# A first expert tile gathered by products with ones, begun beside the ordering of the tiles

## The reference

```python
x = attention(q, k, v)                  # 2 x 8 heads, 768 rows of 64, masked by buckets
P = a0 + a1*h + a2*h**2 + a3*h**3       # h = x @ w_in, 1536 x 2048
y = (P / (1 + |b0|*|h| + |b1|*h**2)) @ w_out
expert = argmax(y @ w_gate)             # 8 experts
gate   = max(softmax(y @ w_gate))
for e in range(8):
    rows = expert == e
    out[rows] = gate[rows] * (relu(y[rows] @ w1[e]) @ w2[e])   # 512 -> 1024 -> 512
```

## Time and profile before

| | us |
|---|---|
| median of three runs | 819.56 |
| lowest and highest run | 818.15, 820.72 |
| the profiled execution: time, and the core's span | 819.36, 817.6 |
| PE busy | 779.0 (95% of the span) |
| DVE, ACT, POOL busy | 564.1, 491.3, 455.6 |
| mean granted TensorE clock | 0.979 |

### The profile page before, as it was taken

The page is one execution under the profiler, slowest core; times in us unless marked ns, Lnnn a source line. Parts: engine busy times, 40 slices in busy tenths (PEclk is TensorE's granted clock), DMA queues, the critical chain, the costliest instruction groups (busy, mean ns, idle before and its releaser), DMA issues.

```text
span 817.6 us, 13322 instructions
## 1 busy us (share of the span) xinstructions
PE 779.0 (95%) x4255; PEld 688.7 (84%) x4255; DVE 564.1 (69%) x967; ACT 491.3 (60%) x973; POOL 455.6 (56%) x404
## 2 busy tenths in 40 slices
PE   6999999999998999999999999994999999999994
PEld 5899899899996889999999999893788888888883
DVE  4788888888896787877788777974454454454451
ACT  4678878878897998778778877944222224223000
POOL 3235265265157688458557644426885659765700
PEclk8899999999999999999999999995999999999998
DMA  9898988985840940950790050074672536460200
GB/s 197 177 209 170 204 173 169 209 168 130 201 148 23 309 160 2 352 176 1 245 375 27 1 206 1 14 259 159 202 239 61 205 133 216 142 234 24 85 14 19
DMA packets 71844, 123.43 MB, mean 151 GB/s; under 512 B 33343, under 2 KB 36127, under 8 KB 67681
## 3 DMA queue, kind: packets, MB, share of 16 engines
q1 hardware_dynamic: 64176, 90.71, 41.3%
q10 hardware_dynamic: 5056, 25.56, 9.4%
q0 software_dynamic: 2544, 6.31, 2.0%
HBM read 60.26 MB, written 34.24 MB: 116 GB/s over the span
## 4 chain that ended last, share of the span: by engine, by line
PE 88%; ACT 5%; DVE 3%; issue 2%; DMA 1%; POOL 1%; SPq 0%; ACTq 0%; POOLq 0%; DVEq 0%
PE ps L1390 7%; PE ps L1478 5%; PE ps L1480 5%; PE ps L1479 5%; PE ps L1512 5%; PE ps L1513 5%; PE ps L1511 5%; PE ps L1656 4%; PE ps L1657 4%; PE ps L1658 4%; PE ps L1682 4%; PE ps L1680 4%; PE ps L1681 4%; PE ps L1378 4%; PE ps L1379 4%; PE ps L1402 4%
## 5 line engine op out<-in xcount | busy, mean ns | idle before, releaser
L786 POOL TENSOR_TENSOR split<-wraw,split 128x512 f32 (+1 forms) x112 | 140.3, 1286 | 54.9 <-ACT split L947 51.4
L947 ACT ACTIVATE split<-wraw 128x512 f32 (+1 forms) x128 | 68.8, 618 | 142.0 <-PE ps L1658 65.9
L1111 DVE TENSOR_TENSOR ptl<-ps,pth 128x512 fp32r<-128x512 f32 x144 | 98.7, 686 | 36.1 <-ACT pth L881 34.1
L761 POOL TENSOR_TENSOR hw<-hw,ha 128x384 f32<-128x384 f32 x64 | 65.4, 1021 | 72.7 <-ACT hw L959 72.7
L881 ACT ACTIVATE pth<-ps 128x512 fp32r<-128x512 f32 x144 | 86.7, 602 | 31.4 <-PE ps L1390 31.3
L1091 DVE TENSOR_REDUCE negmax<-ps 128x1 f32<-128x768 f32 x96 | 91.0, 948 | 8.4 <-PE ps L1379 8.4
L872 ACT ACTIVATE pr<-ps,negmax 128x768 f32<-128x768 f32 x96 | 86.8, 904 | 6.8 <-DVE negmax L1091 6.8
L1390 PE MATMUL ps<-cst,pr 128*128 128x128 f32 x576 | 88.5, 274 | 1.1 <-ACT pr L872 1.1
L1478 PE MATMUL ps<-xh,wih 128*128 128x384 f32 x256 | 86.2, 337 | 1.0 <-DVE hp L1147 1.0
L1480 PE MATMUL ps<-xh,wil 128*128 128x384 f32 x256 | 86.3, 337 | 0.0
L1479 PE MATMUL ps<-xl,wih 128*128 128x384 f32 x256 | 85.9, 336 | 0.0
(11 more groups left out here) (205 smaller groups left out, 2008.9 us busy)
## 6 DMA issues: line engine op xcount, KB each, us to landing
routed<-blank SPq DMA_DIRECT2D x33, 771.0 KB, 13.6
wraw<-in_moe_w ACTq DMA_DIRECT2D x24, 1024.0 KB, 5.4
wraw<-in_moe_w SPq DMA_DIRECT2D x8, 1024.0 KB, 5.4
operand<-qk_hi SPq DMA_DIRECT2D x31, 192.0 KB, 4.2
operand<-qk_hi SPq DMA_DIRECT2D x15, 384.0 KB, 4.7
operand<-qk_lo SPq DMA_DIRECT2D x30, 192.0 KB, 4.3
operand<-mask SPq DMA_DIRECT2D x14, 384.0 KB, 5.0
xg<-routed SPq DMA_DIRECT2D x19, 256.0 KB
```

The costliest lines, as they stand in the source:

```text
L786: pool.tensor_tensor(split_piece(E_LO[x], ring, k), wraw[:, x, i, :], split_piece(E_HI[x], ring, k).bitcast(F32), ALU.subtract).then_inc(e ...
L1111: dve.tensor_tensor(ptl[:, at:at + CW], ps[:, 4 + c % 2, :], pth[:, at:at + CW].bitcast(F32), ALU.subtract).then_inc(ptl_done, 1)
```

## The change

- Blocks 0 to 7 are routed as before. SP then reads slots 0 to 127 back at once (`s_x0`), and POOL's scatters of blocks 8 to 11 wait until that has landed.
- The rows of the blocks 8 to 11 that belong to tile 0 are picked on PE. DVE compares slot numbers with an iota (`picks(j)`), which gives a 128x128 matrix of ones and zeros, and `gather(j)` multiplies the block by it: four matmuls into PSUM bank 5. The read-back rows are added with the identity, four more matmuls, and `xt_ready` is raised.
- `choose` is cut in two: `gate(c)` has the gate values. For c = 2 and 3 it stands later. ACT's turned block 11 comes ahead of exponential 2, and `ranks(2)` ahead of `logit(10)`.
- Four matmuls whose result is not used (`keep_warm(4)`) stand before `gather(9)`.
- ACT copies `xth` of tile 0, between two groups of its weight pieces.
- `mm1` multiplies by `xth` first and by `xtl` after, half by half, and so waits for `xt_hi` only. In tile 0 the last four small products of the ordering stand after its first eight matmuls; `table_done` follows them.
- PE's order for the first tiles: mm1(0), turn_h(0), half of mm2(0), turn_x(1), mm1(1), turn_x(2), the other half of mm2(0), turn_h(1). DVE's follows it.
- `hs` lies ahead of `hth` in memory, an iota of 128 columns is loaded with the constants.

The diff, cut to what the prediction speaks of:

```diff
+            sp.wait_ge(g_done, NSTEP * M4)
+            sp.dma_start(iota[:, :], consts[:, C_IOTA:C_IOTA + P]).then_inc(s_iota, 16)
...
                 sp.dma_start(xg[t % 2][:, :], rows[:, 0:DM]).then_inc(s_xg[t % 2], 16)
+                if t == 1:
+                    sp.wait_ge(xt_ready, 1)
+                    sp.dma_start(gi[:, 0, :], routed[0:P, DM:ROW]).then_inc(s_xg[0], 16)
...
+            sp.wait_ge(s_route, 16 * FIRST_PICK)
+            sp.dma_start(xg[0][:, :], routed[0:P, 0:DM]).then_inc(s_x0, 16)
+            sp.wait_ge(rows_done, 1)
             sp.wait_ge(s_route, 16 * NJ)
-            rows_in(0)
-            sp.wait_ge(rows_done, 1)
...
                 for j in range(CT * c, CT * (c + 1)):
+                    if j == FIRST_PICK:
+                        pool.wait_ge(s_x0, 16)
                     pool.indirect_dma_start(out=routed, ...
...
-            for x in range(2):
-                weights_hi(x, 1, RING_STEP, range(8))
+            weights_hi(0, 1, RING_STEP, range(8))
+            weights_hi(1, 1, RING_STEP, range(4))
+            act.wait_ge(xt_ready, 1)
+            act.activation(xth[:, :, :], ps[:, x_bank(0), :].rearrange("p (k n) -> p k n", n=P), ACT.Copy).then_inc(xt_hi, 1)
+            weights_hi(1, 1, RING_STEP, range(4, 8))
...
+            def picks(j):
+
+                dve.tensor_scalar(pick[:, j - FIRST_PICK, :], iota[:, :], slotf[:, j:j + 1], None, ALU.is_equal).then_inc(pick_done, 1)
...
             choose(2)
             place(2)
+            dve.wait_ge(slot_done, 5)
+            dve.wait_ge(s_iota, 16)
+            picks(8)
+            gate(2)
             choose(3)
             place(3)
+            dve.wait_ge(slot_done, 7)
+            for j in range(9, NJ):
+                picks(j)
...
+            x_in(0)
             dve.wait_ge(seg_pe, 4)
             link(dve.tensor_scalar(tab_need[0:1, :], ...
...
+            relu(0)
+            dve.wait_ge(s_route, 16 * NJ)
+            h_in(0, range(0, 1))
+            x_in(1)
+            h_in(0, range(1, 2))
+            for t in range(1, NSLOT_TILES):
                 relu(t)
...
+            def gather(j):
+
+                pe.wait_ge(pick_done, j - FIRST_PICK + 1)
+                for kt in range(KD):
+                    pe.matmul(ps[:, X0_BANK, kt * P:(kt + 1) * P], y[:, j, kt:DM:KD], pick[:, j - FIRST_PICK, :],
+                              start=(j == FIRST_PICK and kt == 0), stop=False)
+
+            def keep_warm(n):
+
+                some = split_piece(S_W1H, 0, 0)
+                for i in range(n):
+                    pe.matmul(ps[:, 4, :], some[:, 0:P], some, start=True, stop=True)
...
+            ranks(2)
             logit(10)
-            ranks(2)
             logit(11)
+            gather(8)
             ranks(3)
...
+            pe.wait_ge(e_lo[0], 8)
+            keep_warm(4)
+            gather(9)
...
+            pe.wait_ge(s_x0, 16)
+            for kt in range(KD):
+                mm = pe.matmul(ps[:, X0_BANK, kt * P:(kt + 1) * P], xg[0][:, kt:DM:KD], ident, start=False, stop=(kt == KD - 1))
+            mm.then_inc(xt_ready, 1)
...
-                pe.wait_ge(xt_done, t + 1)
+                pe.wait_ge(xt_hi, t + 1)
                 for c in range(2):
                     wait(pe, hs_done, 2 * t - 1 + c)
                     for kt in range(KD):
                         k = KD * c + kt
                         pe.matmul(ps[:, c, :], xth[:, kt, :], weights(S_W1H, t, k), start=(kt == 0), stop=False)
-                        pe.matmul(ps[:, c, :], xtl[:, kt, :], weights(S_W1H, t, k), start=False, stop=False)
-                        mm = pe.matmul(ps[:, c, :], xth[:, kt, :], weights(S_W1L, t, k), start=False, stop=(kt == KD - 1))
+                        pe.matmul(ps[:, c, :], xth[:, kt, :], weights(S_W1L, t, k), start=False, stop=False)
+                    if c == 0:
+                        if t == 0:
+                            last_segments()
+                        pe.wait_ge(xt_done, t + 1)
+                    for kt in range(KD):
+                        mm = pe.matmul(ps[:, c, :], xtl[:, kt, :], weights(S_W1H, t, KD * c + kt), start=False, stop=(kt == KD - 1))
...
-            turn_x(0)
             mm1(0)
+            turn_h(0)
+            mm2(0, range(0, KF // 2))
             turn_x(1)
-            turn_h(0)
             pe.wait_ge(table_done, 1)
-            for t in range(1, NSLOT_TILES):
+            mm1(1)
+            turn_x(2)
+            mm2(0, range(KF // 2, KF))
+            turn_h(1)
+            for t in range(2, NSLOT_TILES):
```

More of the change, by code:

```diff
@@ L248, in build @@
         chosen = put("chosen", [P, E], F32)
+        iota = put("iota", [P, P], F32)
+        pick = put("pick", [P, NJ - FIRST_PICK, P], F32)
         put = Map(csel_at)
@@ L1197, in choose, with gate @@
                     dve.wait_ge(scum_done, j + 1)
+            def gate(c):
+                js = slice(CT * c, CT * (c + 1))
                 dve.wait_ge(ex_done, c + 1)
@@ L1227, in _ @@
             choose(0)
+            gate(0)
             y_add(NSTEP - 1, 0)
@@ L1233, in _ @@
             choose(1)
+            gate(1)
             first_lo_of(1, range(6, 8))
@@ L1254, in _ @@
             dve.scalar_tensor_tensor(out=runs[on, 1:2], in0=upto[on, :], scalar=own(G_TWO), in1=runs[on, 0:1], op0=ALU.is_gt, op1=ALU.add).then_inc(seg_dve, 1)
+            gate(3)
             dve.wait_ge(seg_pe, 1)
@@ L1298, in relu, with h_in @@
                     dve.tensor_scalar(hs[:, c * 512:(c + 1) * 512], ps[:, c, :], 0.0, None, ALU.max).then_inc(hs_done, 1)
-            def h_in(t):
-                for c in range(2):
+            def h_in(t, halves=range(2)):
+                for c in halves:
                     dve.wait_ge(ht_ready, 2 * t + c + 1)
@@ L1617, in _ @@
             pe.matmul(ps[on, 7, 128:128 + NSEG], spread(runs[on, 1:2]), cst[on, C_ID:C_ID + NSEG], start=True, stop=True).then_inc(seg_pe, 1)
+            gather(10)
+            gather(11)
             pe.wait_ge(seg_dve, 2)
@@ L1623, in _, with last_segments @@
             pe.matmul(ps[0:1, 7, 224:224 + NTAB], seg[on, G_RING:G_RING + 1], inside[on, :], start=True, stop=True).then_inc(seg_pe, 1)
[L1624 to L1628 removed]
+            def last_segments():
+                pe.wait_ge(seg_dve, 4)
+                pe.matmul(ps[0:1, 7, 256:256 + NTAB], order[on, 0:1], inside[on, :], start=True, stop=True)
+                pe.matmul(ps[0:1, 7, 288:288 + E], seg[on, G_EXPERT:G_EXPERT + 1], chosen[on, :], start=True, stop=True)
+                pe.matmul(ps[0:1, 7, 288 + E:288 + 2 * E], seg[on, G_RING:G_RING + 1], chosen[on, :], start=True, stop=True)
+                pe.matmul(ps[0:1, 7, 320:320 + E], order[on, 1:2], chosen[on, :], start=True, stop=True).then_inc(seg_pe, 1)
             rings, needs = [0], [8]
@@ L1669, in turn_h, with mm2 @@
                     mm.then_inc(ht_ready, 1)
-            def mm2(t):
-                pe.wait_ge(ht_done, 2 * t + 2)
+            def mm2(t, kts=range(KF)):
+                pe.wait_ge(ht_done, 2 * t + (2 if kts.stop == KF else 1))
                 wait(pe, yo_done, t - 1)
@@ L1676, in mm2 @@
                     pe.wait_ge(e_lo[1], needs[t])
-                for kt in range(KF):
+                for kt in kts:
                     if t == 0:
```

64 lines of the change are left out of this document (34 added, 30 removed).

## The result

The forecast was wrong. Over 20 runs of each, the changed kernel takes 821.59 us in the median (818.04 to 827.52), the kernel before 819.57 (817.70 to 820.72). The ratio is 1.0026 with a 95% interval of 1.0013 to 1.0038: slightly slower, where 816.6 and a range up to 819.4 were forecast. The profiled execution took 820.68 (before 819.36), its span is 818.8, PE is busy for 787.2 us (before 779.0) and the mean granted clock is 0.985 (before 0.979). So PE works more, for the most part at a better clock, and the program does not end earlier.

What follows compares the result with a forecast made beforehand. PE's unbroken work after 580 was taken as the bound, reached through the routing waits. mm1(0) 4.1 us earlier, tile 0 ending 4.7 earlier, less 1.7 for the order, limited by POOL at mm1(3), gave 2.8: 816.6 us, range 812.8 to 819.4.

Steps and rivals of the forecast that it cites:

- the price of the products in front of mm1(0): PE before mm1(0): a gather 1.13 us, read-back products 562.4 to 563.5; with ACT's copy, mm1(0) begins at 564.15, 4.1 earlier.
- The rival in which the clock never falls: From 553 to 562 PE's added products hold the clock: gain 6.8 us, time 812.6, chance 0.13.
- The rest of the front: Before mm1(0): picks 0.3 us each, read-back there by 560.6, later scatters landed at 567.7, ACT's copy 0.60.
- the delay of 0.7: ACT began logit(11) only at 552.05, unexplained; 0.65 us won if that goes, 0.6 taken.
- The end at 572.2: mm1(0) takes 8.1 us from 564.15, clock rising after 4.6 us; the end before was 576.87.
- where 7.1 was taken: From mm1(0)'s end to mm1(1)'s start, through relu, turns, DVE's steps and half of mm2(0): 7.1 us, formerly 2.56.
- The second fall: Rival: clock withdrawn in PE's short work behind mm1(0), costing 5.1 to 5.9 us, time 822.1, chance 0.12.
- The first fall: After routing, the clock falls at 554 while matmuls with 8 to 24 columns run; forecast low up to about 569.
- The sum: At tile 3, mm1(3) begins at 601.3 instead of 604.14: gain 2.8 us, 819.36 to 816.6.
- the 1.7 of the new order: From mm1(0)'s end to mm1(2): 16.6 us instead of 14.9, costing 1.7 of the 4.7 won.
- POOL's 0.3: At mm1(3), POOL's eight pieces of r = 2 ready at 601.3, wanted at 601.15; slack of 7.8 us used up.

Runs made afterwards that it cites:

- the last wait filled: Kernel before plus ten unused matmuls in PE's wait ahead of the last tile's mm2: median 818.28 us, ratio 0.9990.
- the old-order kernel: Changed kernel with the second tile's order as before, mm2(0) in one piece after mm1(1): median 825.94 us, ratio 1.0086 to the kernel before.
- the one with POOL before the table: Changed kernel with POOL's wait for the table moved from the second expert's low parts to the third's: median 837.34 us, ratio 1.0226 to the kernel before.
- the ordering filled: Kernel before plus 37 unused 128x512 matmuls in PE's waits between the last logits and mm1(0): median 821.07 us, ratio 1.0028.

## Why the prediction failed

**The term that was mis-sized.** The forecast missed by 5.0 us. The first step that failed is the price of the products in front of mm1(0): "Into this gap go keep_warm(4), 4 x 0.427 = 1.7, and gather(9), 1.13", then two gathers 2.3 and the read-back rows, all priced by the turns of the earlier trace rows. Start to start, gather(9) takes 559.55 - 557.59 = 1.96, gathers 10 and 11 take 564.38 - 560.35 = 4.03, the read-back products 2.13. That is 0.83 + 1.73 + 1.0 = 3.6 too much, and 567.77 - 564.15 is 3.6. The hint stood in the earlier trace rows: the products of the ordering have `x2` for one matmul in the code, the turns `x1`. In the rows here a `transpose` in the code is one record and a float32 `matmul` is two (the 128x512 ones on the rounded high and low parts are one), even if one of its operands holds only ones and zeros; at the lower clock that is twice the time. With twice the price, the start would have been forecast at 567.8, half a microsecond before that of the kernel before. Leaving the gathers out brought the start forward by 3.2 to 3.9 us, less than the 6.0 that gathers 9 to 11 take, because PE then waits for DVE and the read-back; in the time it gave 2 to 3 of the 5.0. The rival in which the clock never falls had the same fault, worse: it priced a gather at 0.6, and four such products took 2.13 at the higher clock.

**The rest of the front was right.** Picks, read-back, scatters behind it and ACT's copy came as taken. Block 11's copy was not late (550.05). In the trace of before's code with the last wait filled it stands 29.8 after the first turn of `y` for 30.5, so the delay of 0.7 was one execution's; its cause stays open.

**Tile 0.** The end at 572.2 needed a low clock for 4.6 us; without the gathers it came to 572.27, with the clock low up to 568.7. In the changed kernel the clock is back at 565, so the end is 574.0 in spite of the late start; with all four gathers and the four matmuls in place it came back between 563 and 566 in seven of eight traces. That the gathers are what brings it back is not shown. mm1(1) 7.5 us after it, where 7.1 was taken, is the three answers of DVE.

**The second fall.** This is the second step that failed. It was a rival at 0.12, argued against by the earlier trace rows, and it is in 8 of the 12 traces of the changed kernel and its variants, the second trace of the changed kernel among them, and in none of the 5 of the kernel before and its variants. A single trace without it in the last tile was thin evidence: the same wait of 2.7 us has it in both traces of the changed kernel. Its place was also too narrow, since it comes from 566.4 to 569.3, at the copy's wait and the start of mm1(0), as well as in the bits of mm2(0). The price asked (5.1 to 5.9) was too high: it falls for part of the stretch only, 1.7 us each time in all but the old-order kernel and the one with POOL before the table. In the two traces of the changed kernel turn_h of tile 3, measured from the first turn of `y`, is at 94.5 without it and 96.2 with it; before has 94.1 and, in the trace with the last wait filled, 94.6.

**The first fall.** The prediction says that the clock fell at 554 while matmuls with 8 to 24 columns were running. In its own trace PE stood idle from 553.76 to 555.04, so that reading was too quick. Another trace of the same code bears it out: with the last wait filled the clock fell at 548.8, among turns and products of 8 columns, with PE busy for 2.00 of every two us from 538 on.

**The sum.** From trace to trace: mm1(0) starts 0.5 earlier (4.1 forecast) and is 2.4 shorter (6.21 for 8.59; the forecast had 0.5 shorter). From its end to mm1(2) it takes 17.1 where it took 14.9, 2.2 for the 1.7 of the new order. mm1(2) is 0.7 earlier, mm1(3) 0.4 after POOL's 0.3, which was forecast; the last mm2 gives 1.7 away. Yet the first turn of `y`, which no edit touches, was 0.7 earlier in that execution already, so nothing at all is left of the gain at tile 3. When the clock falls again, 1.7 is lost there. At a mean clock of 0.985 the kernel before takes 817.9 to 818.2 and the changed one 820.7 to 821.7. It has that clock or a better one in more of its runs, up to 0.991 (818.04), and a worse one in some (0.973, 827.52). So the ratio is only 1.0026 although PE works 8 us more, and the spread goes from 3 to 9.5 us. The parts do not add up in the runs (half of the gathers out is worth as much as all of them), and no kernel here sets where the clock's falls begin, so a sum to the tenth stays open.

## What to carry to other kernels

Price a float32 product by rows of a float32 product, never by a turn of the same shape: count the records for each matmul in the code first, and look for a row at the clock in question, since these products took as long at either. A start that agrees with the forecast to 0.03 us proves nothing if its terms differ. A stage that trades one long wait for several short ones can lose its clock again, so ask for several traces before calling the clock steady, and fill a wait only where the clock is still high and PE has nothing else to do. A late table or list that releases another engine's long run (here POOL's 16 pieces) uses up slack tiles later.

## What was not expected of the hardware

- A VectorE step on 48x8 values of SBUF took 17.34 us beside GpSimd's run of products and 0.27 without it.
- Four float32 products of 128x128 took 2.23 us at the clock 0.50 and 2.13 at 1.00; four turns 1.13 and 0.63.
- The clock fell at 548.8 in a stretch in which PE had been busy without a break since 538 (the kernel before with the last wait filled).
- From 552 to 564 PE was busy without a break in the changed kernel and the clock stayed at 0.50, with gathers and 128x512 matmuls in it; in the kernel before with the ordering filled, the same held from 550 to 568. The Trainium skill, "TensorE: Matmul & The Clock Gate", section "What's actually happening", ties the full clock to the engine having been busy. These stretches do not agree, as far as the profile's busy time says how busy the array is.
- The clock at one place of one kernel differs between executions: the changed kernel's fall in 568 to 571 is in one of its two traces, worth 1.7 us; the one in the last mm2 is in 8 of 12 traces with that wait empty.
